# Zeroing, scatter and routing steps of a fused attention, MoE and FFN kernel moved between attention and the first expert

## What is computed

```python
noisy_logits = x @ w_gate + np.log1p(np.exp(x @ w_noise)) * noise
top2 = np.argpartition(-noisy_logits, 2, axis=1)[:, :2]
for e in range(E):                      # 8 experts, F = 1024
    for k in range(2):
        mask = top2[:, k] == e
        h = np.maximum(x[mask] @ w1[e], 0.0)
        out[mask] += top2_w[mask, k, None] * (h @ w2[e])
h = out @ w_in                          # F2 = 2048
g = h * np.clip(h + 3.0, 0.0, 6.0) / 6.0
return g @ w_out
```

## Time and profile before

| | before |
|---|---|
| device time, median of 3 runs | 1091.69 us |
| lowest and highest run | 1091.28 and 1094.41 us |
| profiled execution, its own time | 1098.93 us |
| its span | 1097.1 us |
| mean granted TensorE clock | 0.961 of full speed |
| PE busy | 1012.9 us (92%) |
| DVE, ACT, POOL busy | 415.4, 231.9, 414.6 us |
| DMA | 115.21 MB, mean 105 GB/s |

### The profile page before, as it was taken

How to read it: one execution, slowest core, us unless ns; L and a number is a source line. 1 busy time by engine, 2 the same in 40 slices (tenths; PEclk the granted TensorE clock), 3 DMA queues, 4 the chain that set the end, 5 groups by cost and what they waited for, 6 DMA issues and landing times.

```text
span 1097.1 us, 20340 instructions
## 1 busy us (share of the span) xinstructions
PE 1012.9 (92%) x8098; PEld 897.1 (82%) x8099; DVE 415.4 (38%) x885; ACT 231.9 (21%) x537; POOL 414.6 (38%) x277
## 2 busy tenths in 40 slices
PE   6898742999999999999999994999999999999998
PEld 5676631999999989999989983988989989889887
DVE  3576672122222222221313125543544445445343
ACT  4664510111111111111111112111111111111111
POOL 3264454928374664738291915610100101000000
PEclk9999955999999999999999996999999999999999
DMA  8774559625344352626151424210110101100000
GB/s 195 170 177 120 173 183 325 195 85 189 110 147 149 120 170 82 201 77 206 61 174 68 134 68 153 77 39 29 39 49 19 38 29 38 36 12 1 29 1 29
DMA packets 105177, 115.21 MB, mean 105 GB/s; under 512 B 27552, under 2 KB 72608, under 8 KB 105120
## 3 DMA queue, kind: packets, MB, share of 16 engines
q1 hardware_dynamic: 86784, 74.04, 22.9%
q10 hardware_dynamic: 12576, 21.50, 5.8%
q0 software_dynamic: 5760, 18.88, 5.3%
HBM read 76.13 MB, written 38.27 MB: 104 GB/s over the span
## 4 chain that ended last, share of the span: by engine, by line
PE 89%; issue 3%; DVE 3%; DMA 3%; POOL 2%; ACT 1%; ACTq 0%; POOLq 0%; DVEq 0%
PE PS L1430 21%; PE PS L1446 20%; PE PS L1547 18%; PE PS L1531 18%; PE PS L1235 2%; DMA x_sorted<-x_cur,slot_cur 2%; PE PS L1414 2%; PE PS L1315 2%; PE PS L1294 1%; PE PS L1278 1%; POOL x_sorted L623 1%; PE PS L1520 1%; PE PS L1327 1%; PE PS L1256 1%; PE PS L1338 0%
## 5 line engine op out<-in xcount | busy, mean ns | idle before, releaser
L1430 PE MATMUL PS<-xs,W 128*128 128x256 f32 (+1 forms) x1536 | 247.7, 312 | 1.5 <-DVE xs L1079 1.5
L1430 PEld LDWEIGHTS PS<-xs,W 128*128 128x128 f32 x1536 | 238.2, 189 | 12.1 <-issue 2.3
L1446 PE MATMUL PS<-W,hs_room 128*128 128x512 f32 x960 | 244.9, 398 | 0.0
L1547 PE MATMUL PS<-W,gs 128*128 128x512 f32 x864 | 217.4, 396 | 4.1 <-issue 2.5
L1531 PE MATMUL PS<-x2s,W 128*128 128x384 f32 x1152 | 218.4, 339 | 1.5 <-DVE x2s L1155 1.5
L607 POOL TENSOR_TENSOR W<-stage,ones_f 128x1024 fp32r<-128x1024 f32 x76 | 144.6, 1903 | 175.5 <-PE PS L1446 166.7
L1531 PEld LDWEIGHTS PS<-x2s,W 128*128 128x128 f32 x1152 | 202.9, 189 | 9.0 <-issue 1.9
L1446 PEld LDWEIGHTS PS<-W,hs_room 128*128 128x128 f32 x960 | 174.7, 188 | 33.1
L1085 DVE SCALAR_TENSOR_TENSOR hs_room<-PS,hs_room 128x256 fp32r<-128x256 f32 (+1 forms) x128 | 62.8, 491 | 346.0 <-ACT hs_room L771 346.0
L1547 PEld LDWEIGHTS PS<-W,gs 128*128 128x128 f32 x864 | 160.9, 188 | 36.5 <-issue 6.3
L609 POOL TENSOR_TENSOR W<-stage,W 128x1024 fp32r<-128x1024 f32 x76 | 181.7, 2390 | 6.0
(11 more groups left out here) (134 smaller groups left out, 596.4 us busy)
## 6 DMA issues: line engine op xcount, KB each, us to landing
stage<-in_moe_w_dram SPq DMA_DIRECT2D x64, 512.0 KB, 4.4
x_in<-x_sorted ACTq DMA_DIRECT2D x40, 256.0 KB, 4.4
x_sorted<-zeros SPq DMA_DIRECT2D x8, 1280.0 KB, 7.3
y_sorted<-y_sb ACTq DMA_DIRECT2D x40, 256.0 KB, 2.1
vD<-in_v_dram SPq DMA_DIRECT2D x72, 64.0 KB
out_dram<-o_sb SPq DMA_DIRECT2D x18, 256.0 KB, 2.2
stage<-in_moe_w_in_dram SPq DMA_DIRECT2D x8, 512.0 KB, 3.7
stage<-in_moe_w_out_dram SPq DMA_DIRECT2D x8, 512.0 KB, 3.6
```

Of the source, the lines that this page charges most:

```text
L1430: last = nc.tensor.matmul(HP_[:, c % 2, 0:n], W[:, par, 0, b, at:at + P], xs[:, a, kd, rows], start=start, stop=(kd == KD - 1 and (a, b) = ...
L1446: last = nc.tensor.matmul(Y[:, first + t, :], hs[:, c % 2, a, t * P:(t + 1) * P], W[:, par, 1, b, c * DM:(c + 1) * DM], start=(c == 0 and ...
L1547: last = nc.tensor.matmul(OP[:, tt, :], gs[:, c % 2, a, tt * P:(tt + 1) * P], W[:, 1, c // FC, b, at:at + DM], start=(c == 0 and (a, b) == ...
```

## The change

Four things are moved, and nothing is computed differently.

1. **Zeros.** On SP, all zeros wait until every scatter has landed (`x_sent` of the last lot). The order there becomes: `pad(0)`, expert 1's w1 chunks, `pad(1)`, the zeros of `y_sorted`, expert 1's w2 chunks. ACT's loads of the next expert's rows move from c = 3 to c = 6, and its wait for `y_zeroed` from the expert loop's front to `store_y`.
2. **Ranks.** `RANKS_AFTER` is 5 instead of 7, and the parts ahead of it are drawn together.
3. **Scatters.** Tiles 0 to 13 are scattered inside the attention loop (iterations 8 to 20), before it was tiles 0 to 8 (11 to 19).
4. **Splits.** Of expert 0's chunks, 0 to 3 are split in iterations 4 to 7, chunk 4 behind tile 13's scatters, and 5 to 7 behind the last scatter; before, they were split in iterations 5 to 10, 16 and 18.

Also, DVE makes the low halves of expert 0's first three blocks ahead of the tables for the experts, instead of behind them, and PE and ACT wait for these tables (`tabs_ready`) only before part 1 of an expert.

```diff
-    FIRST_AT = (3, 4, 5, 6, 7, 8, 14, 15)
-    SPLIT_AT = (5, 6, 7, 8, 9, 10, 16, 18)
-    SCATTER_AT = (11, 12, 13, 14, 15, 16, 17, 18, 19)
+    FIRST_AT = (2, 3, 4, 5, 7, 9, 11, 13)
+    SPLIT_AT = (4, 5, 6, 7)
+    SCATTER_AT = (8, 9, 10, 12, 13, 14, 15, 16, 17, 18, 18, 19, 19, 20)
...
-    RANKS_AFTER = 7
+    RANKS_AFTER = 5
...
             sp.wait_ge(s_zero, 1)
-            sp.dma_start(y_sorted[FEWEST * P:MOST * P, :]...
-            sp.wait_ge(pads_ready, 1)
-            pad(0, 0, 0)
-            pad(1, 1, 0)
-            load_expert(1)
+            sp.wait_ge(pads_ready, 1)
+            sp.wait_ge(x_sent, sent(NB - 1))
+            pad(0, 0, 0)
+            load_expert(1, 0, QCH)
+            pad(1, 1, 0)
+            sp.dma_start(y_sorted[FEWEST * P:MOST * P, :]...
+            load_expert(1, QCH)
...
-            for T in range(2, TILES + 2):
-                keep_x(T - 2)
-                if T in SCATTER_AT:
-                    scatter(SCATTER_AT.index(T), 0)
+            for T in range(2, TILES + 3):
+                if T < TILES + 2:
+                    keep_x(T - 2)
+                tiles = [t for t in range(len(SCATTER_AT)) if SCATTER_AT[t] == T]
+                for t in tiles:
+                    scatter(t, 0)
                 if T in SPLIT_AT:
                     split_first(SPLIT_AT.index(T))
-                if T in SCATTER_AT:
-                    pool.wait_ge(sc_full, min(T + 2, TILES))
-                    scatter(SCATTER_AT.index(T), 1)
+                if len(tiles) == 1 and T + 2 <= TILES:
+                    pool.wait_ge(sc_full, T + 2)
+                for t in tiles:
+                    scatter(t, 1)
+            split_first(QCH)
             for t in range(len(SCATTER_AT), TILES):
                 for k in range(2):
                     scatter(t, k)
+            for c in range(QCH + 1, SCH):
+                split_first(c)
...
             def store_y(e, j, base):
                 if j == 0:
+                    act.wait_ge(y_zeroed, 16)
...
-                    if c == 3 and not last:
+                    if c == 6 and not last:
                         act.wait_ge(padded[1 - par], 16 * (i + par + 1) + 1)
...
-                for after, parts in ((RANKS_AFTER, (5, 6)), (3, (0,)), (4, (1,)), (5, (2,)), (6, (4,))):
+                for after, parts in ((RANKS_AFTER, (5, 6)), (3, (0,)), (4, (2, 3))):
...
-                for after, part in ((5, 3), (7, 7)):
+                for after, part in ((3, 1), (4, 4), (6, 7)):
...
             def expert(e, par, last=False):
                 for part in range(2):
                     if part == 1:
+                        pe.wait_ge(tabs_ready, 1)
```

More of the change, by code:

```diff
@@ L88, in attention_moe_ffn @@
     EARLY = (1, 2, 3)
-    assert LOTS[0][0] + LOTS[0][1] + RANKS_AFTER - 1 == LOOP[0] + LOOP_TILES + 2 and LOTS[0][1] == most - 1
+    assert LOTS[0][0] + LOTS[0][1] + RANKS_AFTER - 1 == LOOP[0] + LOOP_TILES and LOTS[0][1] == most - 1
     ROOM = N + MAIN
@@ L491, in load_chunk, with load_expert @@
                 sp.dma_start(stage_dst(c, two), src).then_inc(stage_full[c % STAGES], 16)
-            def load_expert(m, first=0):
-                for c in range(first, SCH):
+            def load_expert(m, first=0, end=SCH):
+                for c in range(first, end):
                     if c < QCH:
@@ L737, in _ @@
             for T in range(LAST_IT):
-                for part in range(3):
-                    for n in due(T, 4 + part):
+                for after, part in ((4, 1), (5, 2)):
+                    for n in due(T, after):
                         route(n, part)
@@ L746, in _ @@
                     move_xt(T - 2)
+                for n in due(T, 3):
+                    route(n, 0)
                 if T + 1 < TILES:
@@ L815, in expert @@
                         x_hi(e, PARTS[1][0] + TURN_AT[0].index(c))
+                act.wait_ge(tabs_ready, 1)
                 live = act.value_load(tab_live[0:1, e:e + 1] if isinstance(e, int) else tab_live[0:1, bass.ds(e, 1)],
@@ L840, in _ @@
                 x_hi(0, j)
-            act.wait_ge(tabs_ready, 1)
-            act.wait_ge(y_zeroed, 16)
             with act.Fori(0, E // 2 - 1) as i:
@@ L1049, in _ @@
             route(NB - 1, 6)
[L1050 to L1059, removed]
-            step(nc.vector.tensor_tensor(blk[:, 3], blk[:, 2], blk[:, 1], ALU.subtract))
-            step(nc.vector.tensor_copy(tab_y[:], blk[0:1, 3]))
-            step(nc.vector.tensor_tensor(blk[:, 0], blk[:, 3], room_e[:], ALU.subtract))
-            nc.vector.tensor_tensor(tab_more_y[:].rearrange("p (e t) -> p e t", e=E),
-                                    tab_more[:].rearrange("p (e t) -> p e t", e=E),
-                                    blk[0:1, 0].unsqueeze(2).broadcast_to([1, E, MORE]), ALU.add).then_inc(tabs_ready, 1)
-            pair_wide = [P, 2 * TILES, E - 1]
-            flat = moved[:].rearrange("p k t e -> p (k t) e")
-            step(nc.vector.tensor_scalar(blk[:, 3], blk[:, 1], float(-ROOM), None, ALU.add))
-            step(nc.vector.tensor_tensor(flat, room_e[:, 1:E].unsqueeze(1).broadcast_to(pair_wide),
-                                         slot_x[:].rearrange("p k t -> p (k t)").unsqueeze(2).broadcast_to(pair_wide),
-                                         ALU.is_le))
-            step(nc.vector.tensor_tensor(flat, flat, blk[:, 3, 0:E - 1].unsqueeze(1).broadcast_to(pair_wide), ALU.mult))
-            step(nc.vector.tensor_reduce(shift[:], moved[:], AX.X, ALU.add))
-            step(nc.vector.tensor_tensor(slot[:], shift[:], slot_x[:], ALU.add))
             def x_lo(e, j):
@@ L1371, in iteration @@
             def iteration(T, i=None):
-                lots = due(T, RANKS_AFTER) if i is None else [-1] if T == LOOP[0] + 2 else []
+                lots = due(T, RANKS_AFTER) if i is None else [-1] if T == LOOP[0] else []
                 if T + 1 < TILES:
@@ L1507, in _ @@
                 turn_x(0, j)
-            pe.wait_ge(tabs_ready, 1)
             with pe.Fori(0, E // 2 - 1) as i:
```

24 lines of the change are left out of this document (added).

## The result

| | before | changed |
|---|---|---|
| median | 1091.97 us (1091.28 to 1094.41, 4 runs) | 1081.08 us (1078.78 to 1084.95, 4 runs) |
| ratio | | 0.990, 95% interval 0.9867 to 0.9933 |
| profiled execution | 1098.93 us, span 1097.1 | 1081.28 us, span 1079.5 |

The change makes the kernel faster, by 10.9 us. Forecast were 18.1 us (1073.6, range 1066 to 1084), so the sign and the range held and the size was 7 us too large. The forecast's own range, rival A's 1069 to 1079, did not hold.

The account below looks back on a forecast made before the run. PE was taken to stand idle before the first `hidden` (188.53 us), held by late scatters and loads beside zeros in flight. Terms -19.7 + 1.1 + 0.5 = -18.1 us, taken from 1091.69, gave 1073.6 us, range 1066 to 1084.

Parts of the forecast that it names:

- rival A: The forecast itself: 1073.6 us, own range 1069 to 1079; chance 0.55.
- attention, up to the last `slot_cur`: Attention loop and its tail: loop 2 us longer, last logits 1 us earlier, `slot_cur` ready at 160.8 instead of 163.8.
- `h_lo` of c = 0 behind tables, gates and splits: DVE at the first expert: tables and gate weights mostly hide ahead of `h_lo`; chunk 5's split costs up to 1.5, taken 0.5.
- ACT's wait for `pad(0)`: ACT at c = 1: the pad lands at 182.5, so PE stalls 1.1 us ahead of `project` of c = 2.
- The start of the experts: Ahead of expert 0: scatters and loads finish sooner, first `hidden` at 168.8 instead of 188.5, a gain of 19.7 us.
- The crowding of iterations 5 to 7: Attention loop: lot 0's parts meet the four remaining splits on DVE, +3.5 us, bounds 0 and +7.
- The removed splits in iterations 8 to 10: Attention loop: DVE instructions no longer stretched beside these splits, -4.5 us.
- The +3.2 for scatters beside `turn_qk`: Attention loop: `turn_qk` takes 1.6 us more beside a scatter, in two more iterations than before, +3.2 us.
- Chunk 4's split: Behind tile 13's scatters on POOL: takes 4.3 us and can stretch the chain to `slot_cur` by up to two collisions, 3 us.
- rival E: Slower: ACT stops until `y_sorted`'s late zeros land ahead of `store_y`; whole gain lost from 41 us on, 1096 at 46; chance 0.04.
- B: Attention at its upper bounds (+4) and ACT waiting for `pad(0)` at about 11 us (+4): 1082 us; chance 0.25.
- rival D: POOL: each of ten moved scatters held by DVE work up to 2 us, 20 us in all: 1092, no change; chance 0.03.

Follow-up runs that it names:

- before_third: The kernel before, unedited, run again on the third chip: 1091.26 us (one run).
- after_third: The changed kernel, unedited, run again on the third chip: 1081.39 us, 0.9892 of the kernel before.
- before_again: The kernel before, unedited, run again on the first chip: 1093.85 us (one run).
- after_again: The changed kernel, unedited, run again on the first chip: 1081.57 us, 0.9899 of the kernel before.
- split_waits: The changed kernel, with POOL waiting for the first `h_lo` ahead of splitting chunks 5 to 7: 1089.79 us on the second chip, 0.9922 of before.
- best_a: Changed kernel; chunks 0-5 split in iterations 4, 5, 8, 9, 12, 13, 6-7 behind first `h_lo`; last scatters one iteration earlier, first loads one later: 1066.3 us, 0.9746 of before.
- best_b: best_a, with SP also sending `pad(0)` before the last lot's scatters have landed: 1066.54 us, 0.9762 of before.
- tables_off: The changed kernel, with DVE's last gate weights moved ahead of expert 6 and final slots ahead of expert 7: 1096.96 us, 0.9975 of before.
- splits_quiet: The changed kernel, with expert 0's chunks 0 to 5 split in iterations 4, 5, 8, 9, 12 and 13: 1091.26 us, 0.9926 of before.
- after_zeros_early: The changed kernel, with the zeros back at their old place on SP: 1083.93 us, 0.9912 of before.
- loads_later: The changed kernel, with expert 0's first four weight chunks loaded one iteration later: 1092.75 us on the second chip, 0.9938 of before.
- before_zeros_late: The kernel before, with only the change's later zeros, order of SP and waits on ACT: 1083.3 us, 0.9912 of before.

## Why the prediction was right, and where its size was wrong

Before_third and after_third ran on one chip with an undisturbed attention loop, and their difference can be set against the sum term by term. The last column has before_again and after_again, from the first chip:

| term | forecast | measured, third chip | first chip |
|---|---|---|---|
| attention, up to the last `slot_cur` | -3.0 | +1.9 | -1.9 |
| last `slot_cur` to first `hidden` | -16.7 | -20.4 | -19.9 |
| `h_lo` of c = 0 behind tables, gates and splits | +0.5 | +5.3 | +5.0 |
| `project` of c = 0 and the next `hidden` at the lower clock | 0 | +2.4 | +1.6 |
| ACT's wait for `pad(0)` | +1.1 | 0 | 0 |
| all behind | 0 | +0.1 | +0.3 |
| sum | -18.1 | -10.7 | -14.9 |

The two profiles of the first chip lie 3.9 us further apart than the medians there, 11.0 us, since after_again's was its fastest execution; the third chip's fit its medians within 1 us.

- **The start of the experts** was read rightly. Tile 14's scatter no longer waits for another's landing, ACT issues the third load at 156.1 (forecast 159.8), the last scatter has landed by 170.3 when SP sends `pad(0)` (174.1). The gain at the first `hidden` was forecast as 19.7 us; measured were 18.5 and, on the first chip, 21.8.
- **The mis-sized term** is the one on DVE's tables: "They hide there, but chunk 5's split begins at 172.1: up to 1.5 us. I take 0.5." It was 5.3, plus 2.4 for a slow `project` right behind it, 7.7 us in all, where 0.5 was put. That is nearly the whole miss of 7.4. The other differences (attention 4.9 worse, the start 3.7 better, `pad(0)` 1.1 better) all but cancel, which is luck. Two things were overlooked. The split began at 167.45, as POOL was done sooner, inside the chain of some 20 dependent DVE instructions. And such a chain is not hit once per split: as soon as one instruction comes free, the next stands beside POOL's following one. Three took 1.6 to 2.4 us each instead of 0.2. Without the splits there (split_waits, best_a, best_b) the same instructions take 0.17 and 0.20 us and `project` of c = 0 comes 5.6 to 6.9 us behind the first `hidden`, as before. That is shown by three kernels; tables_off, where the chain was gone and the splits stayed, has 6.9 us as well, and on the other side stand splits_quiet and after_zeros_early, with more stretched instructions and a longer wait (8.07 and 6.45 us).
- **PE restarted slowly.** After 4.1 us of waiting, the first `project` ran its nine matmuls in 4.21 us instead of 2.25, at the lower of the two clocks (1.2 GHz against 2.4): the granted clock was 0.50 from 174.6 to 178.6, and 1.00 from 181.1 on. PE had been busy 3.67 us of the 15 before the first `hidden`, and 4.1 us idle right ahead of `project`. It was so in all profiles with such a wait: 4.21 us behind 4.02 in after_third and in loads_later, 3.89 behind 4.79 in after_again, 4.07 behind 8.07 in after_zeros_early, 4.21 behind 6.45 in splits_quiet. In split_waits `project` of c = 2 took 3.91 us behind 2.17, while waits of 0.26, 0.98 and 1.60 us (best_a, tables_off, before_zeros_late) were followed by 2.37. With no wait there, in before_third, best_a and split_waits, `project` of c = 0 took 2.25 to 2.27. The forecast had no term for it.
- **The wait for `pad(0)`** was priced rightly and yet cost nothing here: it was covered by the late `h_lo`. In before_zeros_late it showed as 1.60 us and in split_waits as 2.17.
- **Attention.** The crowding of iterations 5 to 7 was forecast as +3.5: iteration 7 alone took 10.3 us against 6.8, as parts 2 to 4 met the splits. The removed splits in iterations 8 to 10 gave less than the -4.5 forecast: from tile 6's `x_new` to tile 9's it is 1.6 us less on the third chip (19.2 against 20.8) and 3.3 on the first (18.7 against 21.9). The +3.2 for scatters beside `turn_qk` did not come in the three profiles of the change, where the chain shows 1.09 to 1.32 us a turn; on the second chip turns were stretched (below). Chunk 4's split held two instructions of the chain to `slot_cur`, 2.02 and 2.08 us in after_third; the prediction named this, with up to 3 us, and put nothing in the sum. Up to `slot_cur` the two chips show +1.9 and -1.9, about 0 where -3.0 was forecast; single profiles don't tell it more closely.
- **Tail of the sum.** Zeros late in front of `store_y` (rival E) did not happen: 18.3 us from an issue at 182.17, down at 200.5. POOL waited 3.86 us for a w2 chunk of expert 1, but then stood 12.5 us idle for PE. Of the rivals, B came nearest by its number (1082), but not by its mechanism: attention came out 4.9 us over the forecast on one chip and 1.1 on the other, but the wait for `pad(0)` cost nothing, and what held the experts was DVE.
- **Scatters starved (rival D)** did not happen: the range on POOL is that of before, 956 to 1189 ns, with DVE at work beside them. The stretched instructions are on the other engine. The Trainium skill, "SBUF — State Buffer", section "Who interferes with whom", says that DVE instructions with two SBUF inputs, and copies, casts and tensor-scalar forms, can be held for a whole GpSimd instruction, and reductions never. The traces agree: L1144, L1016, L1018 and L1060 were held to the end of a split's instruction, the reduction L1142 in splits_quiet took 0.42 us between two held ones. Counted by that rule, DVE's chain would have had a larger term than 0.5 in the sum.

## What to carry to other kernels

When a change moves one engine's bulk work earlier, look at what chains of short dependent instructions now stand beside it on its neighbour: here each of POOL's instructions held one of DVE's until it ended, so tables and gate weights of 5 us became 10.6. Two remedies for the same wait are not added but overlap: here each half of the change alone gave 8.7 or 9.3 us, and both 11.0, with intervals that overlap. And a wait that costs nothing may be covered by a worse one; it came out as soon as that was removed, so the last 15 us came only with several edits together.

## What the runs showed of the hardware that was not expected

- The time went with the chip by 7 us: the kernel before had medians of 1092.6, 1099.7 and 1092.7 us. On the second chip iterations 9, 10 and 12 to 14, which have scatters, took 7.6 to 7.7 us in tables_off, against 6.0 to 6.1 in after_again and after_third; iteration 11, without one, took 6.7 and 6.6. And `turn_qk` fell apart into pieces with gaps that the chain calls issue:

```profile
104.17 0.62 PE PS L1247 x21
104.79 0.29 issue
105.08 0.34 PE PS L1247 x5
105.42 0.40 issue
105.82 0.47 PE PS L1247 x13
```

  In the changed kernel's profile the same turn is one piece:

```profile
103.37 1.12 PE PS L1248 x64
```

  Its cause stays open. It goes with scatters, but not on every chip.
- 3072 KB of zeros took 18.3 us to land in the changed kernel and 21.4 in before_zeros_late, with no scatter beside them (but weight loads), and 16.5 with scatters, so nothing suggests that scatters slowed the zeros. The other way round the cost showed: 5.1 and 4.7 us of two waits.
- Not tried: the ranks moved without the scatters, and the scatters without the moved splits. What each of those is worth by itself is open.
